# Pooled keys of an attention and expert kernel in three chunks of 48

## What is computed

```
q_d, k_d, v_d = means over groups of 4 tokens        # 144 of each head
out_d  = softmax(scale * q_d @ k_d.T) @ v_d
out_up = repeat(out_d, 4, axis=2)
scores = where(|i - j| < 4, scale * q @ k.T, -1e9)
out    = out_up + softmax(scores) @ v
h = x @ w_in;  g = h * tanh(softplus(h));  y = g @ w_out   # 512 -> 2048 -> 512
```

## Time and profile before

| | us |
|---|---|
| median of 3 runs | 500.48 |
| lowest, highest | 499.78, 502.88 |
| the profiled execution | 501.3 |
| its span | 499.5 |

### The profile page before, as it was taken

How to read it: one execution, slowest core, us unless ns; L and a number is a source line. 1 busy time by engine, 2 the same in 40 slices (tenths; PEclk the granted TensorE clock), 3 DMA queues, 4 the chain that set the end, 5 groups by cost and what they waited for, 6 DMA issues and landing times.

```text
span 499.5 us, 10589 instructions
## 1 busy us (share of the span) xinstructions
PE 485.7 (97%) x4260; PEld 434.7 (87%) x4260; DVE 230.5 (46%) x469; ACT 204.4 (41%) x434; POOL 119.6 (24%) x188
## 2 busy tenths in 40 slices
PE   7779999999999999999999999999999999999997
PEld 6568888989988998989888999998999898999996
DVE  4854878455544535435534435345255253222221
ACT  3776566645534424535324434244354241211111
POOL 4897814323213213033032022021020210000000
PEclk9989999999999999999999999999999999999999
DMA  7993074133430330520301302101121000100001
GB/s 252 283 378 123 1 243 154 35 98 90 135 106 0 108 105 1 169 80 28 106 2 55 118 1 56 57 1 56 50 70 56 7 17 1 58 6 1 0 1 63
DMA packets 22704, 39.61 MB, mean 79 GB/s; under 512 B 2688, under 2 KB 8576, under 8 KB 22656
## 3 DMA queue, kind: packets, MB, share of 16 engines
q1 hardware_dynamic: 22656, 38.94, 24.8%
HBM read 34.21 MB, written 4.72 MB: 78 GB/s over the span
## 4 chain that ended last, share of the span: by engine, by line
PE 90%; DMA 3%; POOL 2%; SPq 2%; issue 1%; DVE 0%; ACT 0%; POOLq 0%; DVEq 0%
PE banks L699 40%; PE banks L714 39%; PE banks L630 2%; PE banks L649 2%; PE banks L585 2%; PE banks L603 2%; PE banks L614 2%; PE banks L570 2%; DMA v_in<-in_v 2%; DMA k_t<-in_k 1%; DMA w_out_raw<-in_w_out 1%; SPq L318 1%; POOL prob_pool L467 0%; POOL prob L459 0%; POOL v_half L450 0%
## 5 line engine op out<-in xcount | busy, mean ns | idle before, releaser
L925 DVE CAST g_high<-banks 128x384 fp32r<-128x384 f32 x96 | 53.3, 555 | 175.7 <-PE banks L714 130.1
L699 PE MATMUL banks<-x_high,w_in_high 128*128 128x384 f32 x384 | 131.2, 342 | 2.0 <-DVE g_low L927 1.2
L699 PE MATMUL banks<-x_high,w_in_low 128*128 128x384 f32 x384 | 130.1, 339 | 0.0
L1119 ACT ACTIVATE banks<-banks 128x384 f32<-128x384 f32 x96 | 45.4, 476 | 206.4 <-PE banks L699 206.2
L699 PE MATMUL banks<-x_low,w_in_high 128*128 128x384 f32 x384 | 129.8, 338 | 0.0
L714 PE MATMUL banks<-w_out_high,g_high 128*128 128x512 f32 x288 | 114.9, 399 | 0.0
L714 PE MATMUL banks<-w_out_high,g_low 128*128 128x512 f32 x288 | 113.2, 393 | 0.0
L714 PE MATMUL banks<-w_out_low,g_high 128*128 128x512 f32 x288 | 113.1, 393 | 0.0
L459 POOL TENSOR_TENSOR prob<-prob,small 128x432 f32<-128x432 f32 x24 | 22.6, 942 | 256.6 <-DVE small L889 256.6
L699 PEld LDWEIGHTS banks<-x_high,w_in_high 128*128 128x128 f32 x384 | 72.8, 190 | 4.9 <-DVE g_low L927 1.5
L699 PEld LDWEIGHTS banks<-x_low,w_in_high 128*128 128x128 f32 x384 | 72.8, 190 | 3.4 <-issue 0.5
(11 more groups left out here) (70 smaller groups left out, 472.3 us busy)
## 6 DMA issues: line engine op xcount, KB each, us to landing
v_win<-in_v_win SPq DMA_DIRECT2D x24, 256.0 KB, 3.1
v_in<-in_v SPq DMA_DIRECT2D x32, 160.0 KB, 3.8
k_t<-in_k SPq DMA_DIRECT2D x16, 290.0 KB, 4.0
q_t<-in_q SPq DMA_DIRECT2D x24, 192.0 KB, 3.4
out<-stage SPq DMA_DIRECT2D x17, 256.0 KB, 2.1
k_win<-in_k_win SPq DMA_DIRECT2D x20, 216.0 KB, 3.5
w_out_raw<-in_w_out SPq DMA_DIRECT2D x16, 256.0 KB, 5.5
w_in_raw<-in_w_in SPq DMA_DIRECT2D x16, 256.0 KB, 10.0
```

Of the source, the lines that this page charges most:

```text
L699: last = nc.tensor.matmul(hidden[:, g % HB, 0:TB], w, x[:, k, cols], start=(k == 0 and i == 0), stop=(k == KT - 1 and i == 2))
L925: nc.vector.tensor_copy(g_high[:, g % GB], x).then_inc(g_rounded, 1)
L1119: nc.scalar.activation(x, x, ACT.Mish).then_inc(mish_ready, 1)
```

## The change

The 144 pooled keys of a head are taken as three chunks of 48, six for the two heads. Two chunks stand under each other in one tile of 112 rows (0 to 47 and 64 to 111), so that the six chunks need three transposes of 112x128 instead of four of 112x72. The turned probabilities and the pooled v then have 112 rows, and a chunk's product takes 48 rows: it lies in one quarter of the array. `pooled_outputs` now does only the three products of one row half (`part`), and it is called twice for a unit, four times for a two-batch unit. All six products of a tile add up in the same place of one PSUM bank, which both row halves would write. So the second half waits by a new semaphore, `out_begun`, until the first half has ended, and the window products are split by row half too: `window_outputs(n, r)`.

The band's transposes leave out the rows 112 to 127, and stream 112 columns instead of 128. `scores_and_outputs` puts the pooled scores first. v comes in as 112 rows of 1536 bytes per transfer instead of 80 of 2048, and GpSimd's additions have 112 partitions x 192. VectorE clears the 16 unused columns of each chunk once at the start.

```
+def one_batch(n):
+    return slice(0, 1) if two_batches(n) else slice(0, GT)
+def begun(n):
+    return n + 1 + sum(two_batches(m) for m in range(n))
...
-        Q_IN, K_WIN, K_IN, V_IN, V_WIN = [P, TB], [P, W, KW], [P, PAD + S], [VR, 2, POOL, 2 * D], [P, T * 2 * D]
+        Q_IN, K_WIN, K_IN, V_IN, V_WIN = [P, TB], [P, W, KW], [P, PAD + S], [GR, POOL, VC], [P, T * 2 * D]
...
-                        last = nc.tensor.transpose(b[:, 0, P * i:P * (i + 1)],
-                                                   s["prob"][:, 2 * i:2 * i + 2].rearrange("p w k -> p (w k)"), ident)
+                        last = nc.tensor.transpose(b[:, 0, P * i:P * i + GR],
+                                                   s["prob"][0:GR, 2 * i:2 * i + 2].rearrange("p w k -> p (w k)"),
+                                                   ident[0:GR, 0:GR])
...
+                    for i in range(CHUNKS):
+                        last = nc.tensor.transpose(b[:, 1, P * i:P * i + GR], pooled_turn(s, i), ident[0:GR, 0:GR])
...
+                def pooled_outputs(n, tiles, part, first):
+                    s, rows = work(n), slice(WK * part, WK * part + CK)
+                    half, place_of = pooled_of(n, tiles.start)
+                    for h, i in (((0, 0), (1, 2), (0, 1)), ((1, 1), (0, 0), (1, 2)))[part]:
+                        begins = i != 1 if part == 0 else i < 2
+                        last = nc.tensor.matmul(
+                            out_pool(n)[D * h:D * (h + 1)].rearrange("p (r t g) -> p t r g", r=2, t=TP)[:, tiles],
+                            v_pool[rows, half, place_of, D * i:D * (i + 1)],
+                            s["prob_pool_t"][rows, i, tiles].rearrange("p t (r g) -> p t r g", r=2),
+                            start=first and begins, stop=not first and (i != 1 if part == 1 else i > 0))
+                    return last
+                def begin_outputs(n):
+                    pe.wait_ge(prob_copied, 2 * n + 2)
+                    if 1 <= n < AHEAD:
+                        pe.wait_ge(x_split, n)
+                    pe.wait_ge(v_pooled, pair(n) + 1)
+                    pooled_outputs(n, one_batch(n), 0, True).then_inc(out_begun, 1)
+                def window_outputs(n, r):
+                    s, b = work(n), x_out(n)
+                    v_win, keys = inp(n)["v_win"], slice(WK * r, WK * r + KW)
+                    for tp in range(TP):
+                        for c in range(2):
+                            for h in range(2):
...
+                def end_outputs(n):
+                    pe.wait_ge(v_win_loaded[buffer(n)], 16 * times(n))
+                    if not two_batches(n):
+                        window_outputs(n, 0)
+                    pe.wait_ge(out_begun, begun(n))
+                    if AHEAD <= n < UNITS - 1:
+                        pe.wait_ge(pooled_scored, n + 2)
+                    pooled_outputs(n, one_batch(n), 1, False)
+                    last = window_outputs(n, 1)
+                    if two_batches(n):
+                        pooled_outputs(n, slice(1, GT), 1, True).then_inc(out_begun, 1)
+                        window_outputs(n, 0)
+                        pe.wait_ge(out_begun, begun(n) + 1)
+                        last = pooled_outputs(n, slice(1, GT), 0, False)
+                    last.then_inc(out_ready, 1)
...
                 def scores_and_outputs(n):
-                    pooled_outputs(n - 1)
                     pooled_scores(n)
+                    begin_outputs(n - 1)
                     band_scores(n)
-                    window_outputs(n - 1)
+                    end_outputs(n - 1)
```

More of the change, by code:

```diff
@@ L16 @@
 G = S // POOL
-GH = G // 2
-VR = 80
+CK = 48
+CHUNKS = G // CK
+CP = 64
+VC = 3 * D
 REACH = 3
@@ L78, in pair, with two_batches @@
     return HP * batch(n, GT - 1) + n % HP
+def two_batches(n):
+    return batch(n, 0) != batch(n, GT - 1)
+def one_batch(n):
+    return slice(0, 1) if two_batches(n) else slice(0, GT)
+def begun(n):
+    return n + 1 + sum(two_batches(m) for m in range(n))
 def half_slot(n):
@@ L256, in program @@
         prob_pool_copied = sem("prob_pool_copied")
+        out_begun = sem("out_begun")
         out_ready = sem("out_ready")
@@ L447, in pool_v @@
                         pool.wait_ge(out_ready, n - 3)
-                    v4, pooled = inp(n)["v"][0:GH], v_pool[:, n // HP % 2, n % HP]
+                    v4, pooled = inp(n)["v"], v_pool[:, n // HP % 2, n % HP]
                     for u, half in enumerate((pooled, v_half[:])):
-                        nc.gpsimd.tensor_tensor(half, v4[:, :, 2 * u], v4[:, :, 2 * u + 1],
-                                                ALU.add).then_inc(v_halved, 1)
+                        nc.gpsimd.tensor_tensor(half, v4[:, 2 * u], v4[:, 2 * u + 1], ALU.add).then_inc(v_halved, 1)
                     pool.wait_ge(v_halved, 2 * n + 2)
@@ L624, in pooled_outputs @@
                     pe.wait_ge(v_pooled, pair(n) + 1)
[L625 to L634, removed]
@@ L1069, in pooled_exp @@
                     for h in range(2):
-                        last = nc.scalar.activation(s["prob_pool"][:, h], b[0:GR, h], ACT.Exp,
+                        last = nc.scalar.activation(chunks(s)[:, h], b[0:GR, h].rearrange("p (c k) -> p c k", k=CK), ACT.Exp,
                                                     bias=s["bias"][0:GR, h:h + 1], scale=SCALE_POOLED,
@@ L1280 @@
     k_l[:, :, PAD:] = k.reshape(PAIRS, 2, S, D).transpose(0, 1, 3, 2).reshape(PAIRS, P, S)
-    v_in_l = _np.zeros((PAIRS, 2, VR, POOL * 2 * D), _np.float32)
-    v_in_l[:, :, 0:GH] = v.reshape(PAIRS, 2, 2, GH, POOL, D).transpose(0, 2, 3, 4, 1, 5).reshape(
-        PAIRS, 2, GH, POOL * 2 * D)
+    v_chunks = v.reshape(PAIRS, 2, CHUNKS, CK, POOL, D)
+    v_in_l = _np.zeros((PAIRS, 2, GR, 2, VC), _np.float32)
+    for a in range(2):
+        for part in range(2):
+            rows = slice(WK * part, WK * part + CK)
+            phases = slice(2 * a, 2 * a + 2)
+            for i in range(CHUNKS):
+                h, c = divmod(2 * i + part, CHUNKS)
+                v_in_l[:, a, rows, :, D * i:D * (i + 1)] = v_chunks[:, h, c, :, phases]
+    v_in_l = v_in_l.reshape(PAIRS, 2, GR, 2 * VC)
     k_pad, v_pad = (_np.zeros((B, H, REACH + S + REACH, D), _np.float32) for _ in range(2))
```

54 lines of the change are left out of this document (22 added, 32 removed).

## The result

| | before | after |
|---|---|---|
| median, us | 500.83 | 506.72 |
| lowest, highest | 499.78, 502.88 | 505.76, 507.85 |
| runs | 5 | 5 |
| span of the profiled execution | 499.5 | 505.7 |

The ratio of the times is 1.0113, with a 95% interval of 1.0082 to 1.0144. The change makes the kernel slower by 5.9 us, by the profiled spans 6.2. The prediction was 508.4 us, slower, with a range of 501 to 512.

The account below looks back on a forecast made before the run. TensorE, busy for 485.7 of 499.5 us, was taken to bound the kernel. Main stage +6.6 us and start +1.3 gave +7.9 on a median of 500.5, forecasting 508.4 us, range 501 to 512.

Parts of the forecast that it names:

- The turns: Transposes on TensorE: seven of 112 columns take 0.68 us instead of 0.83 per burst, -0.15 us.
- Entry and change of shape: Start of a burst: all products now lie in quarters, so one filling of 0.16 us goes.
- Pooled and window products: Burst products split by row half: +0.45 us in a one-batch burst, +0.50 in a two-batch one.
- a reach of about three records: TensorE reaches past three waiting records, so lower-half products begin three rounds before the upper windows end, 0.18 us.
- the third rival: Products begin strictly in order and two-batch waits cost 0.4 us each; 516 us in all, chance 0.10.
- The deep reach: Rival: TensorE looks past 16 records, so lower-half products begin early; +1.2 us, 501.7 us, chance 0.17.
- The waits for `out_begun`: TensorE's waits for its own result: no cost in one-batch bursts, 0.02 us in two-batch, 0.4 at most.
- The main stage: Bursts and turns of units 4 to 23: +3.6 us one-batch and +3.0 two-batch, together +6.6.
- The start: Outputs of units 2 and 3 ahead of the first expert product: 0.43 + 0.86, +1.3 us.
- I doubled the cost of unit 3's outputs: Start: unit 3 runs at the 1.2 GHz clock level, so its 0.43 us counts as 0.86.
- I costed the gain on GpSimd at nothing: Start: shorter v sums, 766 to about 575 ns, gain nothing, as unit 2's upsample waits on ScalarE anyway.
- The sum against the median: The profiled span's difference, +7.9 us, put on the median of the runs shown: 500.5 to 508.4.

Follow-up runs that it names:

- b_band112: Kernel before with only the band's four transposes cut to 112 columns, leaving out rows 112 to 127; 500.94 us, ratio 1.0009.
- b_scores_first: Kernel before with the pooled scores of a unit put ahead of the previous unit's pooled outputs in each burst; one run, 502.81 us.
- b_rows_apart: Kernel before with eight window products in the upper row half, then eight in the lower, no wait between; 508.35 us, ratio 1.0162.
- b_filled_again: Kernel before with four filler products ahead of unit 3's outputs, same kernel as b_filled, timed again beside a_filled_again; 500.67 us, ratio 0.9997.
- b_filled: Kernel before with four filler products of zeros on TensorE ahead of unit 3's outputs, behind two bare waits; 499.99 us, ratio 0.9974.
- a_filled2: Changed kernel with the same four filler products ahead of unit 3's outputs as b_filled; 506.81 us, ratio 1.0118.
- a_filled_again: Changed kernel with four filler products, same kernel as a_filled2, timed again beside b_filled_again; 506.25 us, ratio 1.0102.
- a_wait_bare: Changed kernel, window products alternating over row halves again, one-batch second pooled group directly behind the first with only the wait between; 508.69 us, ratio 1.0184.
- a_windows_whole: Changed kernel with window products in one piece again, alternating over row halves, behind the wait and second pooled group; 506.48 us, ratio 1.0116.

## Why the prediction was right, and where it was not

**The turns** (predicted -0.15 us): 0.931 to 0.780, -0.151. Right. `b_band112` confirms the rule of two cycles for each streamed column for the band's part (-0.053 for 64 columns less, where the rule gives 0.056), and what is left fits it for the pooled part.

**Entry and change of shape** (0.16): `b_scores_first` measures 0.129 for one change. Right in kind, 0.03 too large.

**Pooled and window products** (+0.45 and, with the wait's 0.02, +0.52): 2.17 - 1.75 = 0.42 and 2.39 - 1.90 = 0.49 in the chains, and the pieces are as forecast: L667 0.87 ("about 0.9"), L646 0.46 ("near 0.5"). The step on which this rested, a reach of about three records, is confirmed by `b_rows_apart`, which changes nothing else: 0.27 where no reach would give 0.48. The chain of after shows it directly too: L646 pieces of the lower row half stand from 165.04 on, while L667 pieces of the upper half go on beside them. With this the strict order of the third rival falls. The Trainium skill (TensorE: Matmul & The Clock Gate, What overlaps and what doesn't) says that matmuls start strictly in program order; these rows show starts in other quarters of the array out of it, and the measurement decides. The deep reach falls as well, which would have left the one-batch bursts unchanged.

**The waits for `out_begun`** (nothing in one-batch bursts, 0.02 in the others, at most 0.4): the chain has no idle time at either. That alone would show little, since the bare wait's 0.303 us hardly shows as idle time. But bare, the second group costs 0.303 us more than it does under cover, so the cover by other products that I claimed is real.

**The main stage** (+6.6): +6.4 from the turn of unit 4 to the end. By the pieces, 12 x (0.42 - 0.15) + 8 x (0.49 - 0.15) = 6.0. The other 0.4 is 0.02 us in each unit (19.80 - 19.51 = 0.29, where burst and turn give 0.27). Most of it lies in the expert products between a turn and the next burst, which take 0.013 to 0.026 us longer behind most turns, and I don't know its cause.

**The start** (+1.3): this term is wrong; the profiled execution has -0.2, and it is most of the 1.7 us by which 508.4 was too high. Two steps failed, and that the error is no larger than 1.5 us owes something to luck, since the 1.2 GHz stretch changes its place from execution to execution. First, I doubled the cost of unit 3's outputs since they had stood at the 1.2 GHz level in the profile of before, and took that level as fixed to the place. The stretches of after show that it moved: the granted clock is 0.50 from 24.9 to 31.3 us, over filler products and unit 1 and 2's work, and 1.00 from 33.4 on. The outputs of unit 3 and the first expert products come 1.8 us later (37.28 against 35.52), and the 21 products then take 3.85 instead of 5.84: 2.0 back. The place of that level isn't fixed to the kernel either: it stands at 0.73 from 24.9 to 31.3 us in `b_filled_again` and at 1.00 in `b_filled`, the same kernel, and at 1.00 in `a_filled2` and 0.50 in the slowest run of `a_filled_again`.

Second, I costed the gain on GpSimd at nothing. The chain of before runs through GpSimd there:

```profile
28.31 0.66 POOL prob_pool L467
...
29.84 1.09 POOL q_halves L429 x2
...
31.45 0.48 PE banks L585 x8
```

and my view of ScalarE had missed it. Its v sums went from 766 to 635 ns (575 by the sum):

```profile
L474 POOL TENSOR_TENSOR v_half<-v_in 112x192 f32<-112x192 f32 x16 | 10.2, 635 | 0.0
```

The pooled transposes of unit 3, which stand ahead of the outputs of unit 2, show who leads, in the timelines of before and of `a_wait_bare`:

```profile
29.12 0.55 PE L614 MATMUL banks<-const,prob_pool 112*72 112x112 f32 x4 [0.69 <-POOL prob_pool L467]
```

```profile
27.05 0.45 PE L637 MATMUL banks<-const,prob_pool 112*128 112x112 f32 x3
```

In six of the eight profiled executions with before's v sums TensorE waits there for GpSimd, for 0.19 to 1.15 us; in none of the six with the new sums does it. So GpSimd held TensorE back before, and doesn't in the changed kernel; in `a_filled2` the chain lies on TensorE there. How much of that reaches the first expert product is another matter. Each output is longer at full clock as said (in `b_filled_again` they take 0.56 + 0.61 = 1.17 us, in `a_filled2` 34.87 - 33.30 = 1.57), which is 0.8 for the two. With the same filler and the clock at 1.00 from 31.3 us on, the first expert product comes at 34.87 in `a_filled2`, and at 34.13 and, its halt taken off, 34.17 in the kernel with before's outputs: 0.7 later, near the 0.86 that the sum gives at full clock. These rows speak for a start that is longer at full clock and for the doubling as the larger error; the later timed comparison, 4.7 to 5.3 us in all where the main stage alone is 6.4, speaks against. No kernel changed the v sums alone, and what the start costs at one clock stays open.

**The sum against the median**: I added the difference to the median of the three runs shown, and the five runs gave +5.9. The forecast (+5.5 to +10) held, at its low end, since nothing came of the start's term.

## What to carry to other kernels

In this kernel, small products in tiles of the array are paid by how many tiles have work within the next few records of the program. A sequence that stays in one row half for sixteen records took 0.75 us where 0.48 stood, although the same number of products for the other half follows. So let the row halves alternate in the innermost loops, and hold a product split that forces them apart against what it saves: here 0.15 us in a turn against 0.42 in a burst. Before a term of a start is doubled for a low clock, ask whether the change, and the next execution, leaves that clock where it was, and read the chain itself for which engine leads there. A difference of 1 us in a start that scatters by 1.75 us between executions can't be told by a handful of runs; look first whether one halt makes the scatter.

## What the runs showed of the hardware that I had not expected

A group of products that waits for TensorE's own result with nothing between costs 0.303 us more than the same group under cover, and the rows show nearly none of it as idle time (0.04 us of "issue"): it is inside the busy pieces of the products around it. Window products that alternate between the row halves in fours instead of ones cost 0.034 us more, and in eights 0.267, where both would cost 0.48 without a reach: the reach takes up most of the first and less than half of the second. TensorE can stand still for 1.7 us inside a group of products that waits for nothing in the program (`b_filled`, `b_scores_first`). The granted clock of the start differs between kernels that differ only in the order of small products (three stretches at the 1.2 GHz level in `a_windows_whole`, one in the changed kernel), but also between executions of one kernel (all at 1.00 in `a_filled2`, 0.50 from 24.9 to 43.1 us in `a_filled_again`), so one profile of each tells nothing of the order's part in it.
